# Clustered attention, experts and MLP on one core: first expert tile from one batch, new order inside an expert tile

## The reference

```python
mask = q_assign[:, :, :, None] == k_assign[:, :, None, :]   # nearest centroid of each row
scores = np.where(mask, scale * q @ k^T, -1e9); attn = softmax(scores); a = attn @ v
x = a.transpose(0, 2, 1, 3).reshape(1536, 512)
logits = x @ w_gate; e_idx = argmax(logits, 1); gate_w = softmax(logits)[e_idx]
eom = sigmoid(x @ w_output_gate)
out[rows of e] = gate_w * eom[:, e] * (relu(x[rows] @ w1[e]) @ w2[e])
h = out @ w_in; g = h * sigmoid(1.702 * h); return g @ w_out
```

## Time and profile before

| what | us |
|---|---|
| time, median of 3 runs | 820.08 (820.08 to 820.62) |
| time of the profiled execution | 819.66 |
| its span | 818.2 |
| PE busy | 757.5 (93%) |
| DVE busy | 427.1 (52%) |
| ACT busy | 370.7 (45%) |
| POOL busy | 164.9 (20%) |

### The profile page before, as it was taken

How to read it: one execution, slowest core, us unless ns; L and a number is a source line. 1 busy time by engine, 2 the same in 40 slices (tenths; PEclk the granted TensorE clock), 3 DMA queues, 4 the chain that set the end, 5 groups by cost and what they waited for, 6 DMA issues and landing times.

```text
span 818.2 us, 12201 instructions
## 1 busy us (share of the span) xinstructions
PE 757.5 (93%) x4181; PEld 650.0 (79%) x4181; DVE 427.1 (52%) x787; ACT 370.7 (45%) x709; POOL 164.9 (20%) x251
## 2 busy tenths in 40 slices
PE   3799999999999984898999999989999999999994
PEld 2699899888898883686888888868888888888883
DVE  4587887888888854266455664453322222222221
ACT  2577777777677822265555665452211111110110
POOL 6123232222634944010101010010000200020001
PEclk8799999999999999798999999999999999999997
DMA  8673552744618336455456454260000100010001
GB/s 177 147 174 77 119 128 68 174 92 93 172 33 201 131 117 168 152 209 220 161 187 232 153 197 148 98 220 0 1 1 0 52 1 0 1 53 1 0 1 51
DMA packets 61180, 86.01 MB, mean 105 GB/s; under 512 B 32561, under 2 KB 34753, under 8 KB 60609
## 3 DMA queue, kind: packets, MB, share of 16 engines
q1 hardware_dynamic: 55440, 74.70, 32.5%
q0 software_dynamic: 3376, 6.35, 2.3%
q10 hardware_dynamic: 2304, 4.20, 1.6%
HBM read 56.01 MB, written 8.79 MB: 79 GB/s over the span
## 4 chain that ended last, share of the span: by engine, by line
PE 76%; SPq 5%; DMA 5%; DVE 4%; ACT 4%; issue 3%; POOL 2%; DVEq 0%; ACTq 0%; POOLq 0%
PE ps L938 16%; PE ps L662 10%; PE ps L953 5%; PE ps L955 5%; PE ps L954 5%; PE ps L735 5%; PE ps L899 3%; PE ps L901 3%; PE ps L900 3%; PE ps L881 3%; PE ps L883 3%; PE ps L882 3%; SPq L389 3%; PE ps L712 3%; PE ps L708 2%
## 5 line engine op out<-in xcount | busy, mean ns | idle before, releaser
L1315 DVE TENSOR_TENSOR pt_l<-ps,pt_h 128x384 fp32r<-128x384 f32 x192 | 105.8, 552 | 41.2 <-ACT pt_h L1042 40.1
L1186 ACT ACTIVATE g<-ps 128x512 f32<-128x512 f32 x48 | 28.7, 598 | 209.2 <-PE ps L938 209.2
L1529 DVE CAST gt_h<-g 128x512 fp32r<-128x512 f32 x48 | 20.5, 427 | 184.4 <-ACT g L1186 184.4
L1042 ACT CAST pt_h<-ps 128x384 fp32r<-128x384 f32 x192 | 92.6, 483 | 42.9 <-PE ps L662 42.8
L662 PE MATMUL ps<-ident,probs 128*128 128x128 f32 x576 | 97.5, 278 | 3.9 <-DVE pt_l L1315 2.4
L1274 DVE TENSOR_REDUCE nmax<-ps 128x1 f32<-128x768 f32 x96 | 91.0, 947 | 7.5 <-PE ps L712 7.5
L1013 ACT ACTIVATE probs<-ps,nmax 128x768 f32<-128x768 f32 x96 | 87.6, 913 | 6.2 <-DVE nmax L1274 6.2
L662 PEld LDWEIGHTS ps<-ident,probs 128*128 128x128 f32 x576 | 70.9, 145 | 18.1 <-DVE pt_l L1315 4.8
L938 PE MATMUL ps<-x2t_h,wl 128*128 128x512 f32 x192 | 74.9, 390 | 2.2 <-DVE wl L1461 2.2
L953 PE MATMUL ps<-wh,gt_l 128*128 128x512 f32 x192 | 74.8, 390 | 0.6 <-DVE wl L1456 0.6
L938 PE MATMUL ps<-x2t_h,wh 128*128 128x512 f32 x192 | 74.7, 389 | 0.0
(11 more groups left out here) (192 smaller groups left out, 1462.8 us busy)
## 6 DMA issues: line engine op xcount, KB each, us to landing
raw<-in_moe_w SPq DMA_DIRECT2D x32, 1024.0 KB, 7.6
ka<-hi_t SPq DMA_DIRECT2D x32, 192.0 KB, 3.9
xg<-xs ACTq DMA_DIRECT2D x16, 256.0 KB, 5.9
raw<-in_moe_w_in SPq DMA_DIRECT2D x4, 1024.0 KB, 6.1
raw<-in_moe_w_out SPq DMA_DIRECT2D x4, 1024.0 KB, 7.1
qn<-in_q SPq DMA_DIRECT2D x16, 192.0 KB, 3.7
kn<-in_k SPq DMA_DIRECT2D x16, 192.0 KB, 3.8
vn<-in_v SPq DMA_DIRECT2D x8, 384.0 KB, 4.9
```

What stands on the lines that cost most here:

```text
L1042: nc.scalar.copy(pt_h[g % 2][:, half * GT:(half + 1) * GT, t3 * P:(t3 + 1) * P], ps[:, 4 + half, 0:GQ].rearrange("p (c n) -> p c n", c=GT) ...
L1315: nc.vector.tensor_tensor(pt_l[g % 2][at_p], ps[:, 4 + half, 0:GQ].rearrange("p (c n) -> p c n", c=GT), pt_h[g % 2][at_p].bitcast(F32), AL ...
```

## The change

Batch 1 is gated in two stages: row tiles 6 to 8 when the last but one group is there, between PE's matmuls, and 9 to 11 after the last one. The first expert tile holds only expert 0's rows of batch 0, at most 128; rows missing to 128 are zeroed by one fill inside attention, and the tile is loaded from `xs` like any other. The rest of expert 0 begins at row 128 of its region (`gap` is added to the positions of its batch 1 rows), so experts have nine segments (`SEG`). The gathers, `is_row`, `find_rows`, `lane` and `region` are gone. SP issues the fills of expert 0 and 1, then fetches tile 1, then the other six fills; ACT's fetches wait for those six. `expert_loop` has three bodies for each expert, its first tile, its second and further ones. A tile on PE is now down, xg transposes, down, h transposes, hidden, down, down, h transposes, hidden, y transposes. w2 is split in an expert's first tile and the next expert's w1 in its second; an expert with one tile splits w1 behind it (`first_of_next`). The last tile's second down stands behind the MLP's first step.

The diff, cut to its core:

```diff
+    STAGES = ((0, T), (T, T + GT), (T + GT, NT))
 expert_loop
...
+                tile(eng.snap(counter) if e else None, e, 0)
                 if e:
                     eng.reg_add(counter, counter, 1)
+                if only is not None:
+                    with eng.If(n < 2):
+                        only(e)
                 with eng.If(n > 1):
+                    tile(eng.snap(counter), e, 1)
+                    eng.reg_add(counter, counter, 1)
+                with eng.If(n > 2):
+                    with eng.Fori(2, n):
+                        tile(eng.snap(counter), e, 2)
 SP
+                if i == PPB + 1:
+                    sp.wait_ge(g_first, 1)
+                    n = sp.value_load(filled[0:1, E:E + 1], min_val=0, max_val=S)
+                    sp.dma_start(xs[bass.ds(n, TILE), :], zeros[:, :]).then_inc(s_first, 16)
...
             fetch_second(0)
+            sp.wait_ge(s_first, 16)
+            sp.wait_ge(s_disp, 16 * T)
+            sp.dma_start(xg[:, :], xs[0:TILE, :]).then_inc(xg_in, 16)
...
             sp.wait_ge(g_tiles, 1)
-            for e in range(E):
-                n = sp.value_load(filled[0:1, e:e + 1], min_val=0, max_val=N)
-                sp.dma_start(xs[bass.ds(n + e * REGION, TILE), :], zeros[:, :]).then_inc(s_fill, 16)
             row = sp.value_load(region_row[0:1, 2:3], min_val=0, max_val=E * REGION)
-            sp.wait_ge(s_fill, 32 + 16 * E)
             sp.wait_ge(s_disp, 16 * NT)
+            for e in range(2):
+                fill(e).then_inc(s_first, 16)
+            sp.wait_ge(s_first, 48)
             fetch(row)
+            for e in range(2, E):
+                fill(e).then_inc(s_fill, 16)
             sp.wait_ge(pv_done, PAIRS * NG)
             fetch_second(1)
 PE
             by_token(lastg - 1, (xn_done, lastg - 1))
+            pe.wait_ge(lo_done, 2 * PAIRS * TPP)
+            tile_transpose(0, bank=5)
             for part in range(GT):
                 values(lastg, 1, 1, 1, part, PAIRS - 1)
+            pe.wait_ge(xtl_done, 1)
+            ranks(1)
             by_token(lastg, (xn_done, lastg))
...
-            for t in range(T):
-                gather(t)
-            ranks(1)
...
-            for t in range(T, NT):
-                gather(t)
...
+            hidden(0, 0, 0)
+            pe.wait_ge(g_row, 2)
+            ranks(2)
+            hidden_transpose(0, 0)
+            hidden(0, 0, 1)
             pe.wait_ge(g_tiles, 1)
...
+                g, ep = p + 1, e if k else e - 1
+                down(p, ep, 0)
+                tile_transpose(g)
+                down(p, ep, 2)
+                hidden_transpose(p, 1)
                 pe.wait_ge(xtl_done, g + 1)
+                hidden(g, e, 0)
+                down(p, ep, 4)
+                down(p, ep, 6)
+                hidden_transpose(g, 0)
+                hidden(g, e, 1)
+                turned(p)
...
-            turned(last)
-            for half in range(2):
-                down(last, E - 1, half)
+            down(last, E - 1, 0)
+            down(last, E - 1, 2)
+            hidden_transpose(last, 1)
...
+                        if m == 0 and c == 2 and f % 8 == 0:
+                            pe.wait_ge(w2_lo, 4 * (E - 1) + 2 + f // 4)
...
-                hidden(0)
+                dense(0)
                 if m == 0:
-                    turned(total, 3)
+                    down(last, E - 1, 4)
+                    down(last, E - 1, 6)
 ACT
             def fetch(row):
+                act.wait_ge(s_fill, 32 + 16 * (E - 2))
                 act.dma_start(xg[:, :], xs[bass.ds(row, TILE), :]).then_inc(xg_in, 16)
...
+                split = split_second if k == 0 else split_first
+                whose = e if k == 0 else e + 1
+                row, ahead_row = row_at(p + 1), region_row_of(g + 1)
+                tile_high(g)
+                fetch(ahead_row)
+                high(p, 1)
+                relu(g, 0)
+                if k < 2:
+                    split(whose, 0)
+                    split(whose, 1)
+                scaled(p)
+                high(g, 0)
+                if k < 2:
+                    split(whose, 2)
+                    split(whose, 3)
+                relu(g, 1)
+                turned_high(p, row)
+            def first_of_next(e):
+                for i in range(4):
+                    split_first(e + 1, i)
...
+            split_second(E, 0)
+            split_second(E, 2)
+            high(last, 1)
+            split_second(E, 1)
+            split_second(E, 3)
 DVE
+            tile_low(0, bank=5)
             choose(1, 0)
             choose(1, 1)
+            inverted(lastg)
             place(1)
-            for t in range(T, NT):
-                find_rows(t)
+            normalised(lastg)
+            choose(2, 0)
+            choose(2, 1)
+            place(2)
...
+                row = row_at(p + 1)
+                tile_low(g)
+                low(p, 1)
+                if k < 2:
+                    split(whose, 0)
+                    split(whose, 1)
+                low(g, 0)
+                if k < 2:
+                    split(whose, 2)
+                    split(whose, 3)
+                turned_low(p, row)
```

More of the change, by code:

```diff
@@ L208, in clustered_attention_moe_mlp @@
         moe.close()
[L209 to L212, removed]
         mlp = ExitStack()
@@ new lines, in hidden @@
+                for c in range(DC):
+                    if half == 0:
+                        pe.wait_ge(w1_lo if e else w0_lo, 4 * (e - 1 if e else 0) + c + 1)
+                    w = slice(c * FE + half * HALF, c * FE + (half + 1) * HALF)
+                    nc.tensor.matmul(ps[:, half, :], xt_l[:, c, :], wh[slot][:, w], start=(c == 0), stop=False)
+                    nc.tensor.matmul(ps[:, half, :], xt_h[:, c, :], wl[slot][:, w], start=False, stop=False)
+                    last = nc.tensor.matmul(ps[:, half, :], xt_h[:, c, :], wh[slot][:, w], start=False, stop=(c == DC - 1))
@@ new lines, in hidden, with hidden_transpose @@
+                last.then_inc(h_ready, 1)
+            def hidden_transpose(g, half):
+                pe.wait_ge(hr_done, 2 * g + half + 1)
+                for c in range(4):
+                    last = tr(ps[:, 2 + half, c * P:(c + 1) * P], h32[:, c * P:(c + 1) * P])
+                last.then_inc(ht_ready, 1)
+            hidden(0, 0, 0)
[3 more added lines that the diff above has]
+            hidden(0, 0, 1)
+            pe.wait_ge(g_tiles, 1)
@@ L940, in hidden, with dense_down @@
                     last.then_inc(h2_ready, 1)
-                def down(f):
+                def dense_down(f):
                     pe.wait_ge(g2_done, FC2 * m + f + 3)
@@ L1169, in _ @@
+            def first_of_next(e):
+                for i in range(4):
+                    split_first(e + 1, i)
+            expert_loop(act, tiles, expert_tile, first_of_next)
             last = act.snap(tiles)
             total = last + 1
-            rows = [row_at(last), row_at(total)]
-            turned_high(last, rows[0])
-            for i in range(4):
-                split_second(E, i)
-            scaled(last)
+            row = row_at(total)
+            split_second(E, 0)
+            split_second(E, 2)
@@ L1187, in _ @@
                     if m == 0 and f == 0:
-                        turned_high(total, rows[1], 3)
+                        scaled(last)
+                    if m == 0 and f == 1:
+                        turned_high(last, row, 3)
                     if m == 0 and f < 8:
@@ L1517, in _, with expert_tile @@
-            expert_loop(dve, tiles, expert_tile)
-            last = dve.snap(tiles)
-            total = last + 1
-            rows = [row_at(last), row_at(total)]
-            turned_low(last, rows[0])
-            for i in range(4):
-                split_second(E, i)
+            def expert_tile(p, e, k):
+                if p is None:
+                    return
+                g = p + 1
+                split = split_second if k == 0 else split_first
+                whose = e if k == 0 else e + 1
+                row = row_at(p + 1)
[9 more added lines that the diff above has]
+                turned_low(p, row)
@@ L1525, in _, with first_of_next @@
+            def first_of_next(e):
+                for i in range(4):
+                    split_first(e + 1, i)
+            expert_loop(dve, tiles, expert_tile, first_of_next)
+            last = dve.snap(tiles)
+            row = row_at(last + 1)
+            split_second(E, 0, 0)
+            split_second(E, 2, 1)
+            low(last, 1)
+            split_second(E, 1, 2)
+            split_second(E, 3, 3)
             for m in range(NMG):
@@ L1531, in _ @@
                     nc.vector.tensor_tensor(gt_l[f % 2][:, :], g32[f % 2][:, :], gt_h[f % 2][:, :].bitcast(F32), ALU.subtract).then_inc(g2_done, 1)
-                    if m == 0 and f == 0:
-                        turned_low(total, rows[1], 3)
+                    if m == 0 and f == 1:
```

(1 more changed line is left out.)

345 lines of the change are left out of this document (145 added, 200 removed).

## The result

The changed kernel takes 815.68 us (median of 10 runs, 813.92 to 818.02) against 820.08 (10 runs, 818.78 to 823.12): a ratio of 0.9944, 95% interval 0.9928 to 0.996. So it is faster, by 4.4 us where 12.6 were forecast. Measured again in two later sets of runs, each with its own runs of the kernel before, it took 810.28 (ratio 0.9889, 0.9873 to 0.9905) and 810.23 (0.9879, 0.9858 to 0.99): 8.3 and 10.0 us. The profiled execution of the first measurement took 814.3, span 812.8.

What follows compares the result with a forecast made beforehand. PE was taken as the bound, busy 757.5 of 818.2 us. Terms 7.0 + 3.6 + 1.3 + 3.3 - 2.0 - 0.3 - 0.3 gave 12.6 us, span 805.6, plus 1.9: 807.5 us; 8-in-10 range 800.5 to 816.

Steps and rivals of the forecast that it cites:

- The boundary, gain 7.0: Between attention and down(0, 4): earlier tile 1, less the wait for six fills, gains 7.0 us (2 to 12).
- I take 4: At the boundary: the xg transfer of tile 1 takes 4 us, with six fills behind it and row_info scatters beside it.
- The lead of xt_l shrinks ... I take 2.0 lost: Within each tile: less PE work covers xt_l, costing 0 to 0.35 us a tile for 14 tiles; 2.0 us charged.
- my sign of being wrong: In the expert loop: the prediction is wrong if the step between tiles is over 13.2 us.
- The partial wait: Rival, xg's transposes to hidden: every tile waits for xt_l; 0.5 us delay costs 5 more (812.5); chance 0.08.
- Jumps, 0.03: Rival, PE's expert loop: seven leaps over unused tile bodies stall 2.4 us each, costing 16.8 us (824); chance 0.03.
- The one leap in the trace does not agree: Argument against the jumps: PE's timeline shows no gap at the leap after expert 1's only tile.
- The one-tile expert, 0.3 lost: After expert 1's only tile: casts and splits delay xt_l by 3.8 us, plus a 2.4 us clock dip; 0.3 us lost.
- Fills hold ACT, 1.0, as a rival 0.13: Before down(0, 4): six fills delay it 1.0 us; as rival, it starts near 337, time 813.5; chance 0.13.
- Weight splits, 1.3: In experts' second tiles: six waits of 0.2 us for DVE's first w2 piece go, gaining 1.3 us.
- End of the loop, 3.3: Around the MLP's start: waits of 0.42, 2.21 and 0.63 us go, gaining 3.3 us, or 2 if a margin fails.
- work done ahead, 3.6: By down(0, 4): down(0, 0..3) is already done, and two dummy transposes over the loop go, gaining 3.6 us.

Runs made afterwards that it cites:

- set 1: First set of follow-up runs, on another chip; here its repeat of the unmodified changed kernel: 810.28 us, ratio 0.9889 to the kernel before.
- set 3: Third set of follow-up runs, on another chip; its repeat of the unmodified changed kernel took 810.23 us, ratio 0.9879 to the kernel before.
- late loads: Changed kernel with ACT doing tile_high ahead of both value loads, the row of x2t loaded only behind relu: 805.11 us, ratio 0.983.
- the two edits that removed it alone: Changed kernel with PE's loop back to two bodies an expert (808.75 us), or with 48 never-executed transposes on PE ahead of the loop (810.01 us).
- the one-tile leap over three bodies: Kernel before, with four bodies of the old tile an expert on PE alone: 829.76 us, ratio 1.0111.
- the shifted kernel: Changed kernel with 48 never-executed transposes on PE ahead of the expert loop, moving its bodies in memory: 810.01 us, ratio 0.9868.
- the best version: Changed kernel with value loads behind tile_high, two bodies on PE, and the next tile's xt_h and xt_l between the splits: 801.39 us, ratio 0.9774.

## Why the prediction was right or wrong

The direction was right and the time lies in the range, but the forecast gain of 12.6 us was nearly three times the 4.4 of the first measurement, and 2.6 to 4.3 us too large against the repeats. The forecast's path, split at three events (dense(0) of the forecast is its span of 805.6 less the 276.7 us that the three profiles take from there to the end):

| us | forecast | first | set 1 | set 3 |
|---|---|---|---|---|
| tile 1 with PE | 320.5 | 324.83 | 322.58 | 322.45 |
| down(0, 4) | 330.8 | 333.67 | 329.72 | 329.93 |
| down(0, 4) to dense(0) | 198.1 | 202.4 | 203.1 | 201.6 |
| span | 805.6 | 812.8 | 809.5 | 808.3 |

Of the 7.2 us by which the first span exceeds the forecast, 2.9 arose ahead of down(0, 4) and 4.3 behind it.

- **The boundary, gain 7.0**: the term was right in the repeats (1 us better) and 2.9 too large in the first measurement. Two errors cancelled in the repeats. "I take 4" for xg was wrong, it took 5.9 to 7.5 us, because of row_info's scatters, and not of the fills named first. Against it PE's half clock ended earlier: I charged it for the whole of hidden(1, 0), and it was over near its start, with matmuls 0.23 us apart again from 329.4 in the first profile and from 327.1 in set 1. From xg to down(0, 4), charged at 10.3 us, it took 7.1 in set 1 and 8.8 with the 1.59 of the fills in the first measurement.
- **"The lead of xt_l shrinks ... I take 2.0 lost"**: the failed step. The 13 steps between y transposes other than the one-tile expert's took 172.6 us in all three profiles (the first: 532.50 - 339.74 - 20.16); the forecast had 13 x 12.94 = 168.2. With late loads they took 168.2. So the steps cost 4.4 us more than charged, and as much goes with the late loads. I had taken a middle between 0 and 4.9 and supported it with a value load of the old kernel that ran beside tile_high's work. The chain above shows what the sum left out. ACT's two loads took 1.5 us, as I had it, but in an expert's first tile the loop's own register work (the counter, and the load of the number of tiles, L343) stands ahead of them, another 1.0 us from the issue of `x2t_h` at 340.45. So `xt_h` began 0.9 us after it could have, where I had 0 to 0.35. The steps that end in a first tile were the long ones, up to 13.7 us against 13.0 in a second tile; my sign of being wrong was 13.2, and the mean was 13.3. The partial wait was a rival with 0.08; it is what happened.
- **Jumps, 0.03**: the mechanism is real for one of the seven leaps that I named. One leap cost 4.8 to 5.3 us of idle time, not 2.4, and the other six nothing; so the kernel did not lose by it. "The one leap in the trace does not agree" was an inference from a leap over a single body. Net it cost little, since the splits behind it would have held PE 4.2 us anyway: in the runs without it the one-tile step is 18.6 to 18.8 us instead of 19.4 to 20.8, so 0.6 to 2.2. By the medians the two edits that removed it alone gained 1.5 and 0.2 us, neither clear of noise.
- **The one-tile expert, 0.3 lost**: the wait, put at 3.8 us, measured 4.2, and the clock dip came. Without the leap the sum (12.94 + 6.2 = 19.1) would have been right to 0.5.
- **Fills hold ACT, 1.0, as a rival 0.13**: 1.59 us in the first measurement, nothing in the repeats, 2.29 in the profile of the late loads. Right as charged, and it varies from one execution to the next.
- **Weight splits, 1.3**: the six waits went, but nothing was gained: even with late loads a pair of tiles (12.76 + 13.04 at best) is no shorter than the 12.78 + 13.03 of before. A wait for `xt_l` in the first tile has taken their place, where DVE's loads stand.
- **End of the loop, 3.3, and work done ahead, 3.6**: right, and together 1 us better: of the 198.1 us forecast 10.8 lie outside the 14 steps, and 9.5 to 9.6 were measured. dense(0) waits for nothing but 0.5 us at a weight load.

The Trainium skill ("Runtime: NRT & Kernel Launch", Instruction fetch mechanics) has it that a taken branch to a target outside the two fetched pages waits for a DMA of the target page. The runs agree in kind: same leap, other place, no stall. The profile's view of the DMA queues in set 1, from 351.4 to 352 us, shows a packet of an instruction queue (columns: packets, MB, share of 16 engines) in the middle of the 5.13 us:

```profile
q1 hardware_dynamic: 119, 0.23, 101.5%
q8 instruction: 1, 0.02, 9.7%
```

**Open.** The first measurement lies 5 us above the repeats, and its ten runs do not overlap with theirs (813.92 and up against 811.08 and down). Its profile shows 1.6 us more for xg than set 1's, a median of 8.7 us for the six fills to land instead of 5.3, 1.59 us behind them, and a wait of 3.51 us for the counts in DVE's routing chain that was 1.86 to 1.90 in all later profiles of these kernels; why on that occasion, no run tells. Why the one-tile leap over three bodies was free in set 3 is open as well. An instruction packet near it ran beside some 55 GB/s of other traffic, those of the two stalls beside some 420; but traffic and place were not varied apart, and in the shifted kernel such a packet ran beside 410 GB/s while PE worked on. That the stall is a fetch of instructions is argued from place and packet; no view shows it as such. Holding the scatters back and waiting late for the fills were not tried together.

## What to carry to other kernels

Before reordering a loop, walk each helper engine's whole queue from its last instruction of the old tile, register loads included: a value load (0.7 us with its register operations) ahead of the operation that PE waits for costs PE what the lead no longer covers, and the loop's own loads stand in the same queue. Put such loads behind that operation, and put what PE needs first between bulk work, not behind it. When a transfer seems slow, hold back one neighbour at a time, and then look at what the held work delays: here the scatters did slow the transfer by 3.3 us, and moving them lost more.

## What the runs showed of the hardware that was not expected

- PE's leap over two tile bodies, 128 matmuls, was free in some layouts of the code and cost 4.6 to 5.3 us of idle time in others, with PE at half clock behind it (0.50 from 355 to 359 us in set 1); 48 transposes that are never executed, placed in front, removed it.
- Beside row_info's scatters (one of 128 rows every 1.26 us) a plain load of 256 KB took 5.6 to 7.5 us from issue to use; without them 2.6. Six fills of 256 KB, issued one after the other, landed in 2.0 to 2.3 us each without them; in the kernel before, two ahead of them took 2.4 and 2.8 and six beside them 5.7 to 7.8.
- After the idle time of 4.2 to 5.3 us at the one-tile expert PE's matmuls were 0.43 us apart, half clock, at once or within 1 us; spread over waits of 0.2 and 0.9 us the same work kept the full clock (1.00 in the window from 332.5 to 386 us of the best version, 0.94 in the changed kernel).
